# Output projection of a fused attention and expert kernel: three split products, or one product in plain fp32

## The chip, the cores and the metric

The kernel runs on one core of one Trainium2 chip. Its time is the device time of one execution in microseconds. Two runs of the kernel before gave 541.42 and 541.78 us, median 541.6 us. The profiled execution took 541.32 us; its trace covers a span of 539.7 us, from the first to the last instruction.

## The reference

Three layers follow each other. B = 2 sequences of 768 tokens are 1,536 rows; the model width is 512.

```python
x = attention(q, k, v)                      # 1536 x 512
g = x @ w_gate ; val = x @ w_val            # 512 -> 1536
x1 = (silu(g) * val) @ w_out                # 1536 -> 512: the projection
skip = x1 @ w_skip ; e = argmax(x1 @ w_gate2)
out = x1 + gate * (relu(x1 @ w1[e]) @ w2[e])   # rows with skip > 0 only, else x1
```

The change touches the third line, the product of h = silu(g) * val (1536 x 1536) with `w_out` (1536 x 512), and what is made ready for it.

## The kernel before, in words

Everything is fp32 in memory. Where the kernel wants near-fp32 precision from the type fp32r, it splits each operand in two: hi is the operand written as fp32r by ScalarE, lo is the operand less hi, and the product is hi*hi + hi*lo + lo*hi: three matmuls for one product. Elsewhere (attention scores, values, the routing logits, the first expert layer) it hands plain fp32 to the matmul. In the trace a matmul on two plain fp32 operands stands as two MATMUL and two LDWEIGHTS records, a matmul on fp32r as one of each.

The program has four stages.

1. Attention, unrolled, to about 80 us.
2. Gate and value products, 12 slices of 128 hidden columns, each of 14 split products (lines 1538 to 1542). VectorE mixes their results (`mix`) and writes h to `h_sb`, 12 tiles of 128 tokens x 12 slices. Its last steps, for slice 11, come in the order of `MIXES`: h0 (tiles 0 to 5), then c21, m1, h1 (tiles 6 to 11).
3. Projection, 12 tiles of 128 tokens (`rows_of_x1`, lines 1635 to 1656). For each of the 12 slices f the stationary operand is the 128 x 128 piece of h, the moving one the 128 x 512 row block of `w_out`; all accumulate in one PSUM bank, two banks in turn. A tile is cut in two halves of six slices (`tile_of_x1`): after the first half come four transposes of the previous tile's result and two small rank products, after the second the four logits products of the previous tile. ScalarE copies the result out (`copy_rows`), VectorE picks the expert (`choose`, `gates`, `rows_of`), SyncE stores the rows, GpSimd scatters them to the experts' lists.
4. Experts: blocks of 96 rows, first layer in plain fp32 (line 1720), second layer split (lines 1737 to 1739).

Each engine works through its instructions in the order written; `pe.wait_ge` and the like wait on semaphores. Around the change:

- ScalarE's `split_wo` (line 908) writes the hi parts of the 12 row blocks of `w_out`. The lo parts are made by GpSimd (line 729, five of them) and VectorE (line 1277, seven).
- ScalarE's `split_h` (line 901) and VectorE's `split_h` (line 1268) write hi and lo of each tile of h, two instructions each per tile, one or two tiles ahead of TensorE, which waits for the count `h_split`.
- SyncE loads `w_out` to `wo_raw` during the last slice of stage 2 (line 472), and the first experts' weights during stage 3 (lines 477 and 485), some of them behind waits on `h_split`.

Of the kernel before, what the change touches and what calls it, by code (L numbers as in the profile page):

```python
# [7 lines left out]
F32 = mybir.dt.float32  # L8
# [43 lines left out]
WO_POOL = 5  # L52
# [70 lines left out]
def build(nc, qT, kT, v, va, vb, sizes, w_gv, w_out, w_route, w1, w2, out):  # L123
    ctx = ExitStack()
    with ctx:
# [43 lines left out]
        hh_hi = place("hh_hi", (P, 2, FT1, P), 1, 0, F32R)  # L169
        hh_lo = place("hh_lo", (P, 2, FT1, P), 1, 12, F32R)  # L170
# [3 lines left out]
        xres = place("xres", (P, 2, ROW), 0, 50.25)  # L174
        y_sb = place("y_sb", (P, DM), 0, 54.5)
        xgT = place("xgT", (P, KD * ET), 0, 56.5)
        past, more = place("past", (P, MAXT, E - 1), 0, 61), place("more", (P, E, ETILES), 0, 62)
        hg_hi, hg_lo = place("hg_hi", (P, FT2 * ET), 0, 64, F32R), place("hg_lo", (P, FT2 * ET), 0, 68, F32R)

        wo_raw = place("wo_raw", (P, FT1, DM), 1, 0)  # L180
        wo_split = place("wo_split", (P, 2, 2, FT1 // 2, DM), 1, 24, F32R)
# [6 lines left out]
        first_hi, first_lo = place("first_hi", (P, FT1, P), 2, 0, F32R), place("first_lo", (P, FT1, P), 2, 6, F32R)  # L188
# [3 lines left out]
        w2_hi = [place(f"w2_hi{u}", (P, FT2, DM), *home, F32R) for u, home in enumerate(((1, 78.25), (1, 24)))]  # L192
        w2_lo = [place(f"w2_lo{u}", (P, FT2, DM), *home, F32R) for u, home in enumerate(((0, 0), (1, 40)))]
# [117 lines left out]
        wo_hi_made = sem("wo_hi_made")  # L311
        wo_by_pool, wo_by_dve = sem("wo_by_pool"), sem("wo_by_dve")
        x_hi_made = sem("x_hi_made")
        h_hi_made = sem("h_hi_made")
        h_split = sem("h_split")
# [88 lines left out]

        def wo_at(f, part):

            return wo_split[:, f // (FT1 // 2), part, f % (FT1 // 2), :]

        @block.sync
        def _(sp):  # L410
# [117 lines left out]
        def _(pool):  # L528
# [1307 lines left out]
```

## Time and profile before

| | |
|---|---|
| median of 2 runs | 541.6 us |
| profiled execution, its span | 541.32 us, 539.7 us |
| TensorE busy (matmul) | 519.0 us, 96% |
| TensorE weight loads busy | 461.5 us, 86% |
| VectorE, ScalarE, GpSimd busy | 318.3, 214.8, 206.8 us |
| granted TensorE clock, mean | 0.99 |
| share of TensorE in the chain that ended last | 89% |

Busy time of TensorE counts an interval once even where several matmuls are in flight, and a matmul's duration is longer than the distance from its start to the next one's, since they are pipelined. What a matmul costs the engine is that distance, and it is read from the start times of a run of equal instructions.

### The profile page before, as it was taken

How to read it: one execution, taken by the hardware profiler on the slowest of the kernel's cores; microseconds unless marked ns; L12 is line 12 of the kernel's file. 1: busy time of each engine (PE TensorE's matmuls, PEld its weight loads, DVE VectorE, ACT ScalarE, POOL GpSimd, SP SyncE). 2: the span in 40 equal slices, each digit the busy share in tenths (PEclk: the TensorE clock that was granted, in tenths of full speed). 3: DMA queues.
4: the chain of work that ended last, by engine and by line, in shares of the span. 5: the costliest groups of instructions: out<-in, count | busy, mean ns of one | idle time of the engine just before them, and what ended most of it. 6: DMA issues, size and time to landing. Idle time of an engine off the chain costs nothing.

```text
span 539.7 us, 11863 instructions
## 1 busy us (share of the span) xinstructions
PE 519.0 (96%) x3889; PEld 461.5 (86%) x3889; DVE 318.3 (59%) x789; ACT 214.8 (40%) x531; POOL 206.8 (38%) x301
## 2 busy tenths in 40 slices
PE   7999996999999999999989999999999999999993
PEld 5777774999999999999968888888888888888882
DVE  5777777777777777777782343743371515451450
ACT  5778762333333333333643333522231313331440
POOL 7255798966565555555500001010221111111111
PEclk9999999899999999999999999999999999999998
DMA  8996520078777777775635111673319855981511
GB/s 235 299 253 205 173 86 22 2 236 250 232 232 226 237 235 246 232 240 179 234 131 224 56 58 58 234 267 122 108 50 348 315 219 173 339 353 31 185 30 29
DMA packets 42471, 99.69 MB, mean 185 GB/s; under 512 B 2737, under 2 KB 15025, under 8 KB 38337
## 3 DMA queue, kind: packets, MB, share of 16 engines
q1 hardware_dynamic: 24784, 61.24, 32.5%
q10 hardware_dynamic: 15088, 29.87, 18.3%
q0 software_dynamic: 2560, 8.09, 4.5%
q8 instruction: 22, 0.36, 0.3%
q14 instruction: 17, 0.13, 0.1%
HBM read 61.11 MB, written 38.07 MB: 184 GB/s over the span
## 4 chain that ended last, share of the span: by engine, by line
PE 89%; DVE 4%; ACT 2%; issue 1%; DMA 1%; POOL 1%; ACTq 0%; DVEq 0%; POOLq 0%
PE bank L1720 14%; PE bank L1538 11%; PE bank L1542 10%; PE bank L1540 10%; PE bank L1650 6%; PE bank L1654 6%; PE bank L1652 6%; PE bank L1526 4%; PE bank L1737 4%; PE bank L1739 3%; PE bank L1738 3%; PE bank L1503 3%; PE bank L1482 3%; PE bank L1670 2%; ACT probs L812 2%
## 5 line engine op out<-in xcount | busy, mean ns | idle before, releaser
L1538 PE MATMUL bank<-x_blocks,w_blocks 128*128 128x384 f32 x336 | 113.4, 338 | 4.3 <-issue 2.2
L1542 PE MATMUL bank<-x_blocks,w_blocks 128*128 128x384 f32 x336 | 113.2, 337 | 0.0
L1540 PE MATMUL bank<-x_blocks,w_blocks 128*128 128x384 f32 x336 | 113.0, 336 | 0.0
L1720 PEld LDWEIGHTS bank<-xgT,w_sb 128*128 128x128 f32 x704 | 80.4, 192 | 1.4 <-issue 0.4
L1720 PE MATMUL bank<-xgT,w_sb 128*128 128x96 f32 x704 | 80.7, 275 | 0.0
L1538 PEld LDWEIGHTS bank<-x_blocks,w_blocks 128*128 128x128 f32 x336 | 63.8, 190 | 5.1 <-issue 5.1
L1540 PEld LDWEIGHTS bank<-x_blocks,w_blocks 128*128 128x128 f32 x336 | 63.8, 190 | 0.0
L1542 PEld LDWEIGHTS bank<-x_blocks,w_blocks 128*128 128x128 f32 x336 | 63.7, 189 | 0.0
L1650 PE MATMUL bank<-wo_split,hh_hi 128*128 128x512 f32 x132 | 53.7, 407 | 1.8 <-issue 1.8
L642 POOL TENSOR_TENSOR w_blocks<-w_sum,w_blocks 128x256 fp32r<-128x256 f32 x48 | 36.2, 755 | 45.4 <-ACT w_blocks L803 45.4
L736 POOL DMA_INDIRECT expert_rows<-x,row_i x12 | 11.9, 990 | 108.7 <-DVE row_i L1339 100.6
L1654 PE MATMUL bank<-wo_split,hh_lo 128*128 128x512 f32 x132 | 51.8, 393 | 0.0
L1652 PE MATMUL bank<-wo_split,hh_hi 128*128 128x512 f32 x132 | 51.4, 389 | 0.0
L812 ACT ACTIVATE probs<-scores_sb,negmax 128x208 f32<-128x208 f32 (+1 forms) x96 | 42.7, 446 | 16.5 <-DVE negmax L1084 16.5
L994 ACT ACTIVATE hg_hi<-bank 128x384 fp32r<-128x384 f32 x22 | 10.8, 491 | 91.5 <-PE bank L1720 91.5
L1382 DVE SCALAR_TENSOR_TENSOR hg_lo<-bank,hg_hi 128x384 fp32r<-128x384 f32 x22 | 12.2, 556 | 56.2 <-ACT hg_hi L994 56.2
L1084 DVE CUSTOM_DVE_ANT_0 scores_sb<-bank,mask 128x208 f32<-128x208 f32 (+1 forms) x96 | 29.2, 356 | 16.5 <-PE bank L1482 13.5
L1347 DVE TENSOR_TENSOR w_lo<-w_raw,w_hi 128x1024 fp32r<-128x1024 f32 x32 | 37.2, 1218 | 2.6 <-ACT w_hi L959 2.6
L803 ACT ACTIVATE w_blocks<-w_sum 128x256 fp32r<-128x256 f32 x48 | 19.8, 413 | 40.2 <-PE bank L1542 37.2
L1737 PE MATMUL bank<-w_hi,hg_hi 128*96 128x512 f32 x88 | 35.5, 403 | 0.0
L1739 PE MATMUL bank<-w_hi,hg_lo 128*96 128x512 f32 x88 | 34.6, 393 | 0.0
L1738 PE MATMUL bank<-w_lo,hg_hi 128*96 128x512 f32 x88 | 34.5, 392 | 0.0
(197 smaller groups left out, 952.4 us busy)
## 6 DMA issues: line engine op xcount, KB each, us to landing
expert_rows<-pad ACTq DMA_DIRECT2D x10, 2891.2 KB, 14.6
w_raw<-w SPq DMA_DIRECT2D x16, 1024.0 KB, 6.3
w_sb<-w SPq DMA_DIRECT2D x16, 1024.0 KB, 8.9
w_raw<-w_gv SPq DMA_DIRECT2D x12, 512.0 KB, 10.5
va_sb<-v_long SPq DMA_DIRECT2D x10, 512.0 KB, 4.0
vb_sb<-v_tail SPq DMA_DIRECT2D x10, 320.0 KB, 5.3
k_sb<-kT SPq DMA_DIRECT2D x12, 256.0 KB, 5.7
wo_raw<-w_out SPq DMA_DIRECT2D x4, 768.0 KB, 6.3
```

The lines of the kernel that those rows point to most:

```text
L812: nc.scalar.activation(probs[:, qt % 2, h * 2 + u, cols], scores_sb[:, i % 4, cols], ACT.Exp, bias=negmax[:, i % 4:i % 4 + 1], scale=-1.0, ...
L1347: last = nc.vector.tensor_tensor(w2_lo[u][:, f:f + FT2 // 4, :].rearrange("p k c -> p (k c)"), w2_raw[:, p, q:q + FT2 // 4, :].rearrange(" ...
L1538: nc.tensor.matmul(ps, wb[:, p, 0, k, :], xb[:, X_OF[p], 0, k, cols], start=(k == 0 and p in (P1, P6, P5, P7)), stop=False, skip_group_che ...
L1540: nc.tensor.matmul(ps, wb[:, p, 0, k, :], xb[:, X_OF[p], 1, k, cols], start=False, stop=False, skip_group_check=True)
L1542: last = nc.tensor.matmul(ps, wb[:, p, 1, k, :], xb[:, X_OF[p], 0, k, cols], start=False, stop=(k == KD // 2 - 1), skip_group_check=True)
L1650: nc.tensor.matmul(out_ps[u][:, :], h_hi, wo_at(f, 0), start=(f == 0), stop=False, skip_group_check=True)
L1652: nc.tensor.matmul(out_ps[u][:, :], h_hi, wo_at(f, 1), start=False, stop=False, skip_group_check=True)
L1654: last = nc.tensor.matmul(out_ps[u][:, :], h_lo, wo_at(f, 0), start=False, stop=(f == FT1 - 1), skip_group_check=True)
L1720: last = nc.tensor.matmul(ps, w1_sb[u][:, k, fc], xgT[:, k * ET:k * ET + ET], start=(k == 0), stop=(k == KD - 1))
L1737: nc.tensor.matmul(y_ps[0:ET, :], hg_hi[:, hf], w2_hi[u][:, f, :], start=(f == 0), stop=False)
L1738: nc.tensor.matmul(y_ps[0:ET, :], hg_hi[:, hf], w2_lo[u][:, f, :], start=False, stop=False)
L1739: last = nc.tensor.matmul(y_ps[0:ET, :], hg_lo[:, hf], w2_hi[u][:, f, :], start=False, stop=(f == FT2 - 1))
```

## The change

All 144 products of the projection (12 tiles x 12 slices) take `h_sb` and `wo_raw` as they are, in plain fp32: one call to matmul for three. ScalarE's, VectorE's and GpSimd's splits of h and `w_out` go, with the buffers `hh_hi`, `hh_lo`, `first_hi`, `first_lo`, `wo_split` and their semaphores. TensorE now waits for the mixing steps h0 and h1 themselves and for the loads of `w_out`. Its loop over tile pairs is unrolled. `xg`, `xres`, the hidden rows of the experts and the second halves of the expert weights move to other places in on-chip memory; the loads of the experts' weights that waited for `h_split` wait for `rows_in_psum`, and GpSimd's first load of `xg` waits for `products_done`.

```diff
-        xg = place("xg", (P, ROW), 0, 48)
+        xg = place("xg", (P, ROW), 1, 24)
...
-        w2_hi = [place(f"w2_hi{u}", (P, FT2, DM), *home, F32R) for u, home in enumerate(((1, 78.25), (1, 24)))]
-        w2_lo = [place(f"w2_lo{u}", (P, FT2, DM), *home, F32R) for u, home in enumerate(((0, 0), (1, 40)))]
+        w2_hi = [place(f"w2_hi{u}", (P, FT2, DM), *home, F32R) for u, home in enumerate(((1, 78.25), (1, 48)))]
+        w2_lo = [place(f"w2_lo{u}", (P, FT2, DM), *home, F32R) for u, home in enumerate(((0, 0), (0, 48)))]
...
                 if t == NT // 2:
-                    sp.wait_ge(h_split, 2 * 6)
+                    sp.wait_ge(rows_in_psum, 6)
                     load_w1(1)
                 if t == NT // 2 + 1:
-                    sp.wait_ge(h_split, 2 * 8)
+                    sp.wait_ge(rows_in_psum, 8)
                     load_w1(2)
...
-            pool.wait_ge(products_done, LAST + DONE_AT[P5, 1])
-            for f in range(WO_POOL):
-                pool.wait_ge(wo_hi_made, f + 1)
-                nc.gpsimd.tensor_tensor(wo_at(f, 1), wo_raw[:, f, :], wo_at(f, 0).bitcast(F32), ALU.subtract
-                                        ).then_inc(wo_by_pool, 1)
-
...
-            pool.wait_ge(h_split, 2 * (NT - 1))
+            pool.wait_ge(products_done, FT1 * PER_F)
...
-            a.wait_ge(w_lo_made, W_BLOCKS * FT1)
-            a.wait_ge(mixed, FT1 * PER_MIX)
-            split_h(0, 0, first_hi, range(1))
-            a.wait_ge(products_done, LAST + DONE_AT[P6, 1])
-            split_wo(0)
-            split_wo(1)
-            a.wait_ge(mixed, FT1 * PER_MIX + MIX_AT["h0", 0])
-            split_h(0, 0, first_hi, range(1, 2))
-            a.wait_ge(products_done, LAST + DONE_AT[P7, 1])
-            split_wo(2)
-            split_wo(3)
...
-                if (name, j) == ("m0", 1):
-                    split_h(0, 0, first_hi, first_lo, range(1))
-                if (name, j) == ("h0", 1):
-                    split_h(0, 0, first_hi, first_lo, range(1, 2))
-                    d.wait_ge(products_done, LAST + DONE_AT[P3, 1])
-                    split_wo(range(WO_POOL, FT1 * 3 // 4))
-                if (name, j) == ("c21", 1):
-                    split_wo(range(FT1 * 3 // 4, FT1))
...
-            def rows_of_x1(t, u, q, fs=None, hi=None, lo=None):
+            def rows_of_x1(t, u, q, fs=None):
 
                 fs = range(q * FT1 // 2, (q + 1) * FT1 // 2) if fs is None else fs
-                pe.wait_ge(h_split, t * 2 + q + 1)
                 if fs[0] == 0:
 
                     pe.wait_ge(x1_ready, t - 1 + FREE_OUT)
+                    if t % (QT // 2) == 0:
+                        pe.wait_ge(mixed, FT1 * PER_MIX + MIX_AT["h0" if t < QT else "h1", t // (QT // 2) % 2])
                 for f in fs:
...
-                    h_hi = hh_hi[:, u, f, :] if hi is None else hi[:, f, :]
-                    h_lo = hh_lo[:, u, f, :] if lo is None else lo[:, f, :]
-                    nc.tensor.matmul(out_ps[u][:, :], h_hi, wo_at(f, 0), start=(f == 0), stop=False,
-                                     skip_group_check=True)
-                    nc.tensor.matmul(out_ps[u][:, :], h_hi, wo_at(f, 1), start=False, stop=False,
-                                     skip_group_check=True)
-                    last = nc.tensor.matmul(out_ps[u][:, :], h_lo, wo_at(f, 0), start=False,
+                    if t == 0 and f % (FT1 // 4) == 0:
+                        pe.wait_ge(wo_in[f // (FT1 // 4)], 16)
+                    last = nc.tensor.matmul(out_ps[u][:, :], h_sb[:, t, f, :], wo_raw[:, f, :], start=(f == 0),
                                             stop=(f == FT1 - 1), skip_group_check=True)
...
-            pe.wait_ge(mixed, FT1 * PER_MIX + MIX_AT["c12", 0])
             for q in range(2):
-                rows_of_x1(0, 0, q, hi=first_hi, lo=first_lo)
+                rows_of_x1(0, 0, q)
             pe.wait_ge(mixed, FT1 * PER_MIX + MIX_AT["c21", 1])
             tile_of_x1(1, 1, first=True)
-            with pe.Fori(1, NT // 2 - 1) as j:
-                tile_of_x1(j * 2, 0)
-                tile_of_x1(j * 2 + 1, 1)
+            for t in range(2, NT - 2):
+                tile_of_x1(t, t % 2)
```

The first place is TensorE at the end of tile 1's first half and in its second half, before (`hh_hi`, `hh_lo` are the split tile of h, `wo_split` the split `w_out`, `ident` the identity of the transposes). The program lists a matmul once, whether the profile has one record of it or two.

```order
L1650 MATMUL bank<-wo_split,hh_hi 128x512
L1652 MATMUL bank<-wo_split,hh_hi 128x512
L1654 MATMUL bank<-wo_split,hh_lo 128x512
L1663 MATMUL bank<-ident,x_78 128x128 [waits x1T_ready,x1_ready]
L1663 MATMUL bank<-ident,x_78 128x128 x3
L1650 MATMUL bank<-wo_split,hh_hi 128x512 [waits h_split]
```

At the same engine the start of the projection in the changed kernel, tile 0 and the first half of tile 1, reads:

```order
L1566 MATMUL bank<-wo_raw,h_sb 128x512 [waits mixed,wo_in0,x1_ready,wr_in]
L1566 MATMUL bank<-wo_raw,h_sb 128x512 x2
L1566 MATMUL bank<-wo_raw,h_sb 128x512 [waits wo_in1]
L1566 MATMUL bank<-wo_raw,h_sb 128x512 x2
L1566 MATMUL bank<-wo_raw,h_sb 128x512 [waits wo_in2]
L1566 MATMUL bank<-wo_raw,h_sb 128x512 x2
L1566 MATMUL bank<-wo_raw,h_sb 128x512 [waits wo_in3]
L1566 MATMUL bank<-wo_raw,h_sb 128x512 x2
L1566 MATMUL bank<-wo_raw,h_sb 128x512 [waits x1_ready,mixed]
L1566 MATMUL bank<-wo_raw,h_sb 128x512 x5
```

Three rows per slice have become one, and the waits on `h_split` have become waits on the mixing and the loads.

The second place is VectorE between the mixing step h0 and its first work for the routing, before:

```order
L1230 TENSOR_TENSOR h_sb<-m_95,m_97 128x3x128 [waits mixed]
L1268 TENSOR_TENSOR first_lo<-h_sb,first_hi 128x768 [waits h_hi_made]
L1277 TENSOR_TENSOR wo_split<-wo_raw,wo_split 128x512 [waits wo_hi_made,products_done]
L1277 TENSOR_TENSOR wo_split<-wo_raw,wo_split 128x512 [waits wo_hi_made] x3
L1255 TENSOR_TENSOR c_96<-bank,u_93 128x384 [waits products_done] x2
L1277 TENSOR_TENSOR wo_split<-wo_raw,wo_split 128x512 [waits wo_hi_made] x3
L1258 TENSOR_TENSOR m_97<-m_97,c_96 128x384 [waits sig_ready]
```

The same stretch in the changed kernel:

```order
L1180 TENSOR_TENSOR h_sb<-m_92,m_94 128x3x128 [waits mixed]
L1205 TENSOR_TENSOR c_93<-bank,u_90 128x384 [waits products_done] x2
L1208 TENSOR_TENSOR m_94<-m_94,c_93 128x384 [waits sig_ready]
L1180 TENSOR_TENSOR h_sb<-m_94,v_mix 128x3x128 [waits mixed]
L1208 TENSOR_TENSOR m_94<-m_94,c_93 128x384 [waits sig_ready]
```

The step c21 (`c_96`, now `c_93`), for which TensorE waits before tile 1, has lost the lo parts that stood ahead of it.

## Rows read from the trace of the kernel before

**Rows 1.** The page, part 1: busy time, share of the span, instructions.

```profile
PE 519.0 (96%) x3889; PEld 461.5 (86%) x3889; DVE 318.3 (59%) x789; ACT 214.8 (40%) x531; POOL 206.8 (38%) x301
```

**Rows 2.** Windows: stretch, its length, busy us of each engine, PEclk, DMA share, GB/s.

```profile
268.50:276.70 8.20, 8.20 (x38) 6.59 (x36) 8.16 (x13) 4.42 (x9) 0.97 (x1) 1.00 0.00 0
276.70:278.60 1.90, 0.18 (x1) 0.00 (x0) 1.83 (x4) 1.90 (x4) 0.00 (x0) 1.00 0.13 26
278.60:390.00 111.40, 111.36 (x591) 94.14 (x592) 46.77 (x185) 36.73 (x75) 12.03 (x13) 1.00 0.41 152
390.00:400.00 10.00, 9.87 (x69) 8.09 (x68) 8.06 (x30) 4.77 (x7) 1.52 (x2) 1.00 0.14 46
400.00:531.00 131.00, 131.00 (x926) 113.81 (x924) 51.81 (x67) 36.84 (x55) 20.28 (x32) 1.00 0.57 209
```

**Rows 3.** Timeline of TensorE, tile 0 and the idle time behind it: start, us.

```profile
268.52 0.39 PE L1650 MATMUL bank<-wo_split,first_hi 128*128 128x512 f32 x1
276.49 0.39 PE L1654 MATMUL bank<-wo_split,first_lo 128*128 128x512 f32 x1
278.64 0.47 PE L1650 MATMUL bank<-wo_split,hh_hi 128*128 128x512 f32 x1 [1.76 <-issue]
```

**Rows 4.** Timeline of TensorE, one tile in the middle of the projection.

```profile
311.89 0.60 PE L1663 MATMUL bank<-ident,x 128*128 128x128 f32 x4
316.60 0.96 PE L1670 MATMUL bank<-wr_sb,x1T 128*128 128x9 f32 x8
317.42 0.47 PE L1650 MATMUL bank<-wo_split,hh_hi 128*128 128x512 f32 x1
317.73 0.39 PE L1652 MATMUL bank<-wo_split,hh_hi 128*128 128x512 f32 x1
321.63 0.60 PE L1663 MATMUL bank<-ident,x 128*128 128x128 f32 x4
```

**Rows 5.** Timeline of TensorE, plain fp32 score products in attention, cut at three windows.

```profile
20.28 0.41 PE L1482 MATMUL bank<-k_sb,q_sb 64*64 64x208 f32 x4
20.28 0.76 PE L1482 MATMUL bank<-k_sb,q_sb 64*64 64x208 f32 x12
20.28 0.94 PE L1482 MATMUL bank<-k_sb,q_sb 64*64 64x208 f32 x16
```

**Rows 6.** Single lines of the kernel: duration ns min/median/max, first and last start.

```profile
L1482 PE MATMUL bank<-k_sb,q_sb x16: 335/336/387, 20.3 to 20.9; 64*64 64x208 f32 x16
L1526 PE MATMUL bank<-probsT,va_sb x16: 220/222/271, 19.2 to 19.9; 128*64 128x64 f32 x16
L1652 PE MATMUL bank<-wo_split,hh_hi x100: 387/389/395, 299.7 to 379.5; 128*128 128x512 f32 x100
L1540 PE MATMUL bank<-x_blocks,w_blocks x97: 334/334/335, 200.1 to 250.0; 128*128 128x384 f32 x97
```

**Rows 7.** Critical chain in the expert stage: start, us, what.

```profile
414.14 7.12 PE bank L1720 x64
```

**Rows 8.** Lines by form: busy us, mean ns, idle before; TensorE.

```profile
L1720 PEld LDWEIGHTS bank<-xgT,w_sb 128*128 128x128 f32 x704 | 80.4, 192 | 1.4 <-issue 0.4
L1670 PE MATMUL bank<-wr_sb,x1T 128*128 128x9 f32 x88 | 10.5, 247 | 0.0
```

**Rows 9.** Lines by form, VectorE: the split of h.

```profile
L1268 DVE TENSOR_TENSOR hh_lo<-h_sb,hh_hi 128x768 fp32r<-128x768 f32 x22 | 20.0, 953 | 9.6 <-ACT hh_hi L901 9.5
```

**Rows 10.** Timeline of VectorE at the start of the projection.

```profile
266.19 0.56 DVE L1230 TENSOR_TENSOR h_sb<-m,m 128x384 f32<-128x384 f32 x1
270.21 2.49 DVE L1277 TENSOR_TENSOR wo_split<-wo_raw,wo_split 128x512 fp32r<-128x512 f32 x4
272.62 1.01 DVE L1255 TENSOR_TENSOR c<-bank,u 128x384 f32<-128x384 f32 x2
```

**Rows 11.** Timeline of SyncE's queue, and DMA issues: KB each, us to landing.

```profile
256.23 4.02 SPq L472 DMA_DIRECT2D wo_raw<-w_out  x4
wo_raw<-w_out SPq DMA_DIRECT2D x4, 768.0 KB, 6.3
```

More of the change, by code:

```diff
@@ L51 @@
 W_BLOCKS = 7
-WO_POOL = 5
 W_SPLITS = {4: (0, 1), 5: (2, 3), 6: (4,), 7: (5,), 8: (6,)}
@@ L168, in build @@
         all_sum = place("all_sum", (P, 4, KD // 2, P), 2, 26)
-        hh_hi = place("hh_hi", (P, 2, FT1, P), 1, 0, F32R)
-        hh_lo = place("hh_lo", (P, 2, FT1, P), 1, 12, F32R)
         x1 = place("x1", (P, 2, ROW), 1, 72)
         x1T = place("x1T", (P, DM), 1, 76.125)
-        xg = place("xg", (P, ROW), 0, 48)
[L174 to L178, printed above, removed]
+        xg = place("xg", (P, ROW), 1, 24)
+        xres = place("xres", (P, 2, ROW), 1, 26.25)
+        y_sb = place("y_sb", (P, DM), 1, 30.5)
+        xgT = place("xgT", (P, KD * ET), 1, 32.5)
+        past, more = place("past", (P, MAXT, E - 1), 1, 37), place("more", (P, E, ETILES), 1, 38)
+        hg_hi, hg_lo = place("hg_hi", (P, FT2 * ET), 1, 40, F32R), place("hg_lo", (P, FT2 * ET), 1, 44, F32R)
         wo_raw = place("wo_raw", (P, FT1, DM), 1, 0)
-        wo_split = place("wo_split", (P, 2, 2, FT1 // 2, DM), 1, 24, F32R)
         w_raw = place("w_raw", (P, 2, 2, KD, P), 2, 0)
@@ L895, in _ @@
                     slice_of_h(f, u, j * 16 + 16)
-            def split_h(t, u, hi=None, qs=range(2)):
-                for q in qs:
-                    fs = slice(q * FT1 // 2, (q + 1) * FT1 // 2)
-                    nc.scalar.activation((hh_hi[:, u, fs, :] if hi is None else hi[:, fs, :]).rearrange("p f c -> p (f c)"),
-                                         h_sb[:, bass.ds(t, 1), fs, :].rearrange("p a f c -> p (a f c)"),
-                                         ACT.Copy).then_inc(h_hi_made, 1)
-            def split_wo(i):
-                a.wait_ge(wo_in[i], 16)
-                for f in range(i * FT1 // 4, (i + 1) * FT1 // 4):
-                    nc.scalar.activation(wo_at(f, 0), wo_raw[:, f, :], ACT.Copy).then_inc(wo_hi_made, 1)
             copy_p1(FT1 - 1)
             first_sigmoids(FT1 - 1)
-            a.wait_ge(w_lo_made, W_BLOCKS * FT1)
-            a.wait_ge(mixed, FT1 * PER_MIX)
-            split_h(0, 0, first_hi, range(1))
-            a.wait_ge(products_done, LAST + DONE_AT[P6, 1])
-            split_wo(0)
-            split_wo(1)
-            a.wait_ge(mixed, FT1 * PER_MIX + MIX_AT["h0", 0])
-            split_h(0, 0, first_hi, range(1, 2))
-            a.wait_ge(products_done, LAST + DONE_AT[P7, 1])
-            split_wo(2)
-            split_wo(3)
             second_sigmoid(FT1 - 1, 0)
@@ L975, in _ @@
                     copy_rows(t - 1, 1 - u, (j + u) * 16)
-                    split_h(t + 1, 1 - u)
                     exp_logits(t - 2, u)
@@ L1262, in mix @@
                 last.then_inc(mixed, 1)
-            def split_h(t, u, hi=None, lo=None, qs=range(2)):
-                for q in qs:
-                    fs = slice(q * FT1 // 2, (q + 1) * FT1 // 2)
-                    d.wait_ge(h_hi_made, t * 2 + q + 1)
-                    nc.vector.tensor_tensor((hh_lo[:, u, fs, :] if lo is None else lo[:, fs, :]).rearrange("p f c -> p (f c)"),
-                                            h_sb[:, bass.ds(t, 1), fs, :].rearrange("p a f c -> p (a f c)"),
-                                            (hh_hi[:, u, fs, :] if hi is None else hi[:, fs, :]).rearrange(
-                                                "p f c -> p (f c)").bitcast(F32),
-                                            ALU.subtract).then_inc(h_split, 1)
-            def split_wo(fs):
-                for f in fs:
-                    d.wait_ge(wo_hi_made, f + 1)
-                    nc.vector.tensor_tensor(wo_at(f, 1), wo_raw[:, f, :], wo_at(f, 0).bitcast(F32), ALU.subtract
-                                            ).then_inc(wo_by_dve, 1)
             with d.Fori(0, FT1 - 1) as f:
@@ L1360, in _ @@
                     t = j * 2 + u
-                    split_h(t + 1, 1 - u)
                     gates(t - 2, u)
@@ L1365, in _ @@
             for t in range(NT // 2, NT + 1):
-                if t + 1 < NT:
-                    split_h(t + 1, (t + 1) % 2)
                 gates(t - 2, t % 2)
```

21 lines of the change are left out of this document (removed).

## The prediction

> **What bounds the kernel now.** I read the page's busy times first, then the windows by stage, then the timeline of TensorE inside the projection. The busy times show one engine at 96% and the next at 59% [rows 1]. The windows show where that average is made: from 278.6 to 390 us TensorE is busy for 111.36 of 111.40 us, from 400 to 531 us for all of it, and VectorE and ScalarE are busy for less than half of these stretches [rows 2]. The projection begins at 268.52 us, and its only idle time is one gap of 1.76 us behind tile 0 [rows 3]. So in the stage that is changed a microsecond of TensorE is a microsecond of the kernel, and work taken from the other engines is worth at most the 1.8 us of that gap.
>
> The timeline of a middle tile shows how a tile is made up: four transposes at 311.89 and again at 321.63, so 9.74 us per tile, with eight logits records at 316.60 between the halves [rows 4].
>
> **The split products that go.** Tile 0 has 36 wide matmuls with nothing between them; the first starts at 268.52 and the last at 276.49, 35 distances in 7.97 us, 0.2277 us each [rows 3]. The second half of the middle tile gives the same: from the second matmul at 317.73 to the transposes at 321.63 are 17 distances in 3.90 us, 0.229 us [rows 4]. The projection has 12 x 36 = 432 of them: 432 x 0.2277 = 98.4 us, all on the path.
>
> **The plain products that come.** There are 144, and each is two records in the profile, for that is how this kernel's plain fp32 matmuls stand in it: line 1720 has 704 records [rows 8], which are 11 blocks of 32 products, twice. So 288 instructions, 128 rows by 512 columns. No such form is in the trace; the nearest are these.
>
> - The score products in attention, plain fp32, 208 columns, each on a quarter of the array (64 rows, 64 columns). Three cuts of their timeline hold 4, 12 and 16 records that began at 20.28 and last 0.41, 0.76 and 0.94 us [rows 5]. They go four at a time, one on each quarter: from 4 to 12 is two such batches in 0.35 us, from 12 to 16 one in 0.18. From 4 to 16 it is 0.53 / 3 = 0.177 us for a batch, 0.85 ns for a column.
> - The durations of single records say the same in another way. For plain fp32, 222 ns at 64 columns and 336 at 208: 114 / 144 = 0.79 ns per column. For fp32r, 334 at 384 and 389 at 512: 55 / 128 = 0.43 ns per column [rows 6]. So one plain record takes about twice as long per column as one fp32r record. At a granted clock of 1.00 [rows 2], the 2.4 GHz level, these are two periods a column and one.
> - The first expert layer: 64 plain records in 7.12 us, 0.111 us each for 96 columns [rows 7], 1.16 ns per column. But records of 9 columns come eight in the 0.82 us from 316.60 to 317.42, 0.103 us each [rows 4]. So that distance hardly depends on the columns; it is the load of the 128 x 128 weights, whose records fill 80.4 us of that layer [rows 8]. Under a matmul of 512 columns such a load is hidden.
>
> The first two give 0.79 x 512 = 0.405 and 0.85 x 512 = 0.436 us for 512 columns; two periods of the 2.4 GHz clock per column are 0.427. I take 0.43 us, with a few ns for the start of each. The bounds are, below, the distance of an fp32r matmul of the same 512 columns, 0.2277 us; above, 1.16 ns x 512 = 0.593 us.
>
> So 288 x 0.43 = 123.8 us in place of 98.4: **+25.4 us**. A product costs 0.86 us where it cost 0.683.
>
> The first wide matmul behind logits or transposes takes 0.31 us to the next, 0.08 more than the others [rows 4], because the short records ahead of it cannot hide its weight load. That is the same before and after: two per tile, no difference.
>
> **A rule on the same price.** The rows above put the two records of a product at four column periods. The Trainium skill (FP8 and Floating Point Precision, TensorE Precision Notes) says that true fp32 makes four passes through the array, which speaks against replacing three; the durations agree in kind. If each pass cost what an fp32r matmul costs here, a product would be 4 x 0.2277 = 0.911 us, and the sum +32.8 instead of +25.4; that case is a rival below.
>
> **The gap behind tile 0.** TensorE waits there, at 276.7, for the split of tile 1, which ScalarE starts only when the lo parts of `w_out` are done. All that goes. What is left ahead of tile 1 is the step c21; it ran at 272.62, behind 2.49 us of lo parts that go too [rows 10]. Tile 0 itself now ends at 268.5 + 24 x 0.43 = 278.8. The gap closes: **-1.8 us**.
>
> **New waits, at nothing.** Tile 0 now waits for h0 rather than c12: the first h0 ran from 266.19 to 266.75 [rows 10], before TensorE is free at 268.52. It waits for `w_out` itself: the four issues go out between 256.23 and 260.25 and land after 6.3 us, so by about 266.6 [rows 11]. If that load were late by 3 us, TensorE would stand for one. Tiles 3, 6 and 9 wait for mixing steps that are over by 278. Behind a waiting matmul all of TensorE stands, but none of these is late.
>
> SyncE's loads of the second and third experts' weights stand behind the stores of tiles 6 and 7, by when rows of 7 and 8 tiles are in PSUM, so their new waits are satisfied when reached. Its loads ahead of them go out earlier (the first waits for the last mixing step, the second for the end of tile 0). GpSimd's load of `xg` keeps its place behind the scatter of tile 8, and its new wait is long over. In the expert stage TensorE is busy 131.00 of 131 us [rows 2]; nothing there is shortened, nothing waits.
>
> **Splits that go, at nothing.** The lo parts of h are 22 instructions, 20.0 us of VectorE [rows 9], with ScalarE's hi parts beside. They lie beside TensorE, which waits for none of them after tile 1. VectorE is busy 46.8 of 111.4 us [rows 2]. What they gain is slack.
>
> **Sum.** +25.4 - 1.8 = +23.6 us on the profiled execution's 541.3: 564.9 us. The median of the runs is 0.3 above that execution, within what runs differ by, so I predict **565 us**.
>
> **Rivals.**
>
> *A plain record takes one period per column.* Then 512 columns cost the 0.2277 us of the fp32r matmul, 288 x 0.2277 = 65.6 us, and the kernel gains 32.8 + 1.8 = 34.6 us: 507 us. The place is every wide matmul of the projection; it decides the sign as soon as the distance is below (98.4 + 1.8) / 288 = 0.348 us. For it: the batches of four in attention could in truth be pairs in fast succession. Against it: the durations per column, 0.79 against 0.43 ns, and cuts that hold 4, 12 and 16 records, never 6 or 10. By the Trainium skill (TensorE: Matmul & The Clock Gate, Back-to-back issue gap) the gap of a warm matmul is N / 2.4 + 2.5 ns, with no word on the type; for two records of 512 that would be 0.43 us a product and give this same case. The attention rows speak against reading it so, 0.177 us for 208 columns where it has 0.089. Chance 3%.
>
> *Each plain record or pass carries the extra that fp32r matmuls carry.* 512 columns at 0.43 ns are 0.220 us, and the distance is 0.2277, 8 ns more (14 against bare periods). With 14 ns per record a distance is 0.441, the sum +28.6 - 1.8: 568 us. With four full passes, 572.3 us. For it: no row has plain fp32 with 128-column weights behind wide matmuls. Against it: the batches of 208 columns have 4 ns over two periods a column, not 14. Chance 10%, mostly for the near end.
>
> *The weight load is not hidden*, since each product now loads the same piece of h twice and each record reads at the rate of the first expert layer: 0.593 us, +72.4 - 1.8, 612 us. Against it: a load record lasts 0.192 us [rows 8] and would sit under 0.43. Chance 2%.
>
> *The change is slower on TensorE, but relief elsewhere pays for it*, landing within 2%: it would need 13 us of waits inside the projection or behind it, and the windows hold 0.04 us from 278.6 to 390 and 0.13 from 390 to 400 [rows 2]. Chance 2%.
>
> **Chances and range.** The forecast has 83%. Two per cent of the time is 10.8 us, so slower by over 2% is above 552.4: the forecast, the second and the third rival, 95%. Faster by over 2% is the first, 3%; within 2% the last, 2%. Within the forecast the distance may be 0.42 to 0.44, which is 288 x 0.01 = 2.9 us to each side, and contention may add or take 1 us. The range that holds 8 in 10 is 561 to 570; it takes in the near end of the second rival and leaves out the rest.
>
> **What the changed profile would show.** The distance of two wide records in tile 0: 0.42 to 0.44 us if right, 0.23 or 0.59 for the first and third rival. Tiles at a period of 9.74 + 12 x 0.177 = 11.9 us. No idle time of TensorE behind tile 0, tile 0 starting at 268.5. The expert stage as long as before, shifted. I would be wrong if the plain fp32 rate of attention's quarter-array products did not carry over to the full array, or if tile 0 started late for want of `w_out`.

## The result and the profile after

The changed kernel takes 564.6 us (two runs, 564.46 and 564.80), 1.0425 times the kernel before, 95% interval 1.038 to 1.047. It is slower by 23 us, where +23.6 had been forecast. Its profiled execution took 564.8 us and spans 563.2.

First the page of the changed kernel: busy times, the shares of TensorE and others in the chain that ended last, and the wide matmuls (busy us, mean ns | idle before).

```profile
PE 544.6 (97%) x3745; PEld 436.1 (77%) x3745; DVE 292.4 (52%) x758; ACT 191.7 (34%) x495; POOL 200.2 (36%) x296
...
PE 94%; DVE 2%; issue 1%; ACT 1%; POOL 1%; ACTq 0%; DVEq 0%; POOLq 0%
...
L1566 PE MATMUL bank<-wo_raw,h_sb 128*128 128x512 f32 x288 | 129.0, 598 | 0.0
```

TensorE has 144 records fewer than in [rows 1] (432 went, 288 came) and is busy for 25.6 us more. All other engines are relieved: VectorE by 25.9 us, ScalarE by 23.1, GpSimd by 6.6. None of that shows in the time.

The same stretches as in [rows 2]: each has its length, then the busy us of PE, PEld, DVE, ACT and POOL, the granted clock, DMA share, GB/s.

```profile
268.50:279.00 10.50, 10.50 (x30) 5.24 (x29) 3.35 (x7) 1.05 (x2) 0.00 (x0) 1.00 0.51 197
279.00:414.00 135.00, 135.00 (x466) 70.64 (x465) 29.41 (x165) 24.57 (x57) 12.03 (x13) 1.00 0.30 111
414.00:424.00 10.00, 10.00 (x67) 8.01 (x66) 8.32 (x29) 5.12 (x7) 1.51 (x2) 1.00 0.13 46
424.00:555.00 131.00, 130.65 (x922) 113.43 (x920) 51.30 (x66) 36.49 (x55) 20.56 (x32) 1.00 0.57 209
```

TensorE is never idle in the projection; the gap behind tile 0 is gone, and 130.65 of 131 us of the expert stage are filled (131.00 before), at the same granted clock. The list of TensorE's waits from 269 to 555 us is empty.

The timeline of TensorE at the start of the projection, a tile in its middle, and the first expert matmul:

```profile
269.48 15.61 PE L1566 MATMUL bank<-wo_raw,h_sb 128*128 128x512 f32 x36
284.93 0.60 PE L1575 MATMUL bank<-ident,x 128*128 128x128 f32 x4
...
296.56 0.60 PE L1575 MATMUL bank<-ident,x 128*128 128x128 f32 x4
...
308.33 0.60 PE L1575 MATMUL bank<-ident,x 128*128 128x128 f32 x4
...
409.45 1.11 PE L1630 MATMUL bank<-xgT,w_sb 128*128 128x96 f32 x8
```

The 36 records of tile 0 and the first half of tile 1 now stand as one group. The last of them lasts 0.592 us, so 35 distances take 15.61 - 0.592 = 15.02 us, 0.4291 each. From transposes to transposes is 308.33 - 296.56 = 11.77 us, where [rows 4] had 9.74. The difference of 2.03 us is 12 x (2 x d - 3 x 0.2294), where 0.2294 is the fp32r distance in that tile, 3.90 / 17 [rows 4]; it gives d = 0.4287, the same distance in the middle as at the start.

The account of the two profiled executions, in us, with the stages cut at the first wide matmul and at the first matmul of the first expert layer:

| | before | after | difference |
|---|---|---|---|
| to the start of the projection | 268.52 | 269.48 | +0.96 |
| projection | 117.39 | 139.97 | +22.58 |
| from there to the end of the span | 153.8 | 153.8 | 0.0 |

The first line lies in code that the change leaves as it is. Stage 2 starts at 86.78 us before and 87.75 after, and in the profiles of the experiments below anywhere from 86.27 to 88.69: one execution differs from the next by that much there, so the 0.96 us are not the change's.

### The profile page after: what moved, and what is told of

Read it like the earlier page. It is cut to its first block, busy times and chain, and to the rows that moved or that the text cites. A ratio compares the mean times of both kernels' runs of the same rounds, so it can differ in the third digit from the quotient of the medians.

```text
span 563.2 us, 11433 instructions
## 1 busy us (share of the span) xinstructions
PE 544.6 (97%) x3745; PEld 436.1 (77%) x3745; DVE 292.4 (52%) x758; ACT 191.7 (34%) x495; POOL 200.2 (36%) x296
## 4 chain that ended last, share of the span: by engine, by line
PE 94%; DVE 2%; issue 1%; ACT 1%; POOL 1%; ACTq 0%; DVEq 0%; POOLq 0%
PE bank L1566 22%; PE bank L1630 14%; PE bank L1458 10%; PE bank L1460 10%; PE bank L1462 10%; PE bank L1647 4%; PE bank L1649 4%; PE bank L1648 4%; PE bank L1446 4%; PE bank L1423 3%; PE bank L1402 3%; PE bank L1582 2%; PE bank L1416 1%; PE bank L1575 1%; PE bank L1619 1%
## 5 line engine op out<-in xcount | busy, mean ns | idle before, releaser
L1566 PE MATMUL bank<-wo_raw,h_sb 128*128 128x512 f32 x288 | 129.0, 598 | 0.0
L1566 PEld LDWEIGHTS bank<-wo_raw,h_sb 128*128 128x128 f32 x288 | 53.0, 190 | 57.9 <-issue 57.9
L1229 DVE TENSOR_SCALAR computes<-bank 128x1 f32<-128x1 f32 x12 | 1.9, 157 | 70.9 <-PE bank L1582 68.7
## 6 DMA issues: line engine op xcount, KB each, us to landing
w_raw<-w_gv SPq DMA_DIRECT2D x12, 512.0 KB, 10.5
```

The source lines that it names most:

```text
L1566: last = nc.tensor.matmul(out_ps[u][:, :], h_sb[:, t, f, :], wo_raw[:, f, :], start=(f == 0), stop=(f == FT1 - 1), skip_group_check=True)
```

## The experiments

Three theories were to be told apart first. **Theory A**, that of the prediction: TensorE's stream of columns is the whole story; a plain fp32 record takes two periods of the 2.4 GHz clock per column and next to nothing besides, and relief of the other engines is worth nothing. **Rival B**: each record carries a fixed extra as an fp32r matmul does (0.2277 us against 0.2133 for 512 bare periods, 14 ns). **Rival C**: something of the 23 us is made elsewhere, or was given back elsewhere. The ratios are to the kernel before, timed beside each.

### Two matmuls of 256 columns for one of 512

```diff
-                    last = nc.tensor.matmul(out_ps[u][:, :], h_sb[:, t, f, :], wo_raw[:, f, :], start=(f == 0),
+                    for c in (slice(0, DM // 2), slice(DM // 2, DM)):
+                        last = nc.tensor.matmul(out_ps[u][:, c], h_sb[:, t, f, :], wo_raw[:, f, c], start=(f == 0),
```

> The changed kernel with each plain fp32 product of 512 columns cut into two of 256, same stationary piece of h: 576 records where there were 288, half as wide. If a record costs two clock periods per column and a few ns (0.4286 us at 512 columns in the changed kernel), the distance at 256 columns is about 0.2155 us, 576 x 0.2155 = 124.1 us against 123.4, and the kernel takes 565 us (564.6 + 0.7). If instead a record's cost does not depend on its columns, because the load of its weights or a fixed cost bounds it, 576 x 0.4286 = 246.9 us and the kernel takes 688 us. If the distance has a large fixed part beside the columns, it lands between.

Measured: 604.0 us, ratio 1.116 (1.114 to 1.118), which fits none of the figures expected. But the projection took 409.02 - 268.33 = 140.69 us, only 0.72 more than in the changed kernel; the time is lost behind it. Two lines of its page, matmuls by form:

```profile
L1567 PE MATMUL bank<-wo_raw,h_sb 128*128 128x256 f32 x576 | 129.8, 382 | 0.0
...
L1631 PE MATMUL bank<-xgT,w_sb 128*128 128x96 f32 x896 | 102.6, 275 | 0.0
```

The first expert layer has 896 records, 14 blocks of 64, where it had 704, 11 blocks. Both halves of a PSUM bank began with `start`, and the second `start` made the first slice's part of the left half vanish: the logits came out different, the rows fell to the experts in another way, and three more blocks were needed. The total is 604.0 - 564.6 = 39.4 us above the changed kernel's, so with the 0.7 of the projection taken off, a block costs 12.9. So this kernel leaves a twelfth of the sum of half the columns out, and its total says nothing on the question; its projection does. The same with one `start` per bank:

```diff
-                        last = nc.tensor.matmul(out_ps[u][:, c], h_sb[:, t, f, :], wo_raw[:, f, c], start=(f == 0),
+                        last = nc.tensor.matmul(out_ps[u][:, c], h_sb[:, t, f, :], wo_raw[:, f, c], start=(f == 0 and c.start == 0),
```

> The run with two 256-column halves again, with the accumulation begun once per bank (only the left half of slice 0 clears it), so that the first slice's part of the left half is kept and the experts get the same blocks of rows as in the changed kernel. Two periods per column: 576 records at the 0.216 us that the first version of this run showed are 124.4 us against 123.4, and the kernel takes 564.6 + 0.7 = 565.3 us. A cost per record would give 688 us.

Measured: 564.5 us, ratio 1.043 (1.040 to 1.046), as the uncut changed kernel. Its timeline, the records of tile 0 and half of tile 1, and the durations of its line, ns min/median/max:

```profile
268.55 15.70 PE L1567 MATMUL bank<-wo_raw,h_sb 128*128 128x256 f32 x72
```

```profile
L1567 PE MATMUL bank<-wo_raw,h_sb x576: 378/379/463, 268.6 to 409.0; 128*128 128x256 f32 x192
```

71 distances take 15.70 - 0.379 = 15.32 us, 0.2158 each. Two distances and two widths give the price apart: (0.4291 - 0.2158) / 256 = 0.833 ns per column, exactly two periods of 2.4 GHz, and 0.2158 - 0.2133 = 2.5 ns for a record. The projection takes 409.24 - 268.55 = 140.69 us, again 0.72 more than uncut, and 288 more records of 2.5 ns are 0.72. Rival B wanted 14 ns each, 4 us; it is out.

The Trainium skill (TensorE: Matmul & The Clock Gate, Back-to-back issue gap) has N / 2.4 + 2.5 ns for an isolated warm matmul of N columns. With 2N in the place of N it gives 0.2158 and 0.4292 us for these records, and the trace agrees to 0.1 ns, though these stand in a stream, for which the section expects less than the formula; as it stands it would be short by half.

### The splits put back on ScalarE and VectorE, with nobody waiting for them

```diff
+            def split_h(t):
+                for q in range(2):
+                    fs = slice(q * FT1 // 2, (q + 1) * FT1 // 2)
+                    a.wait_ge(dummy_lo, t * 2 + q)
+                    nc.scalar.activation(dummy[:, fs, :].rearrange("p f c -> p (f c)"),
+                                         h_sb[:, bass.ds(t, 1), fs, :].rearrange("p a f c -> p (a f c)"),
+                                         ACT.Copy).then_inc(dummy_hi, 1)
```

VectorE has the like, a subtraction behind `dummy_hi`, 22 instructions on each engine for tiles 1 to 11.

> The changed kernel with the splits of h given back to ScalarE and VectorE as idle work: tiles 1 to 11 are copied to a scratch buffer and subtracted there, 22 instructions of about 0.84 us on ScalarE and 22 of about 0.95 us on VectorE at the places where they stood; TensorE reads neither and waits for neither. If the relief of these engines is worth nothing in the projection, the kernel takes 564.6 us again, within 1. If part of the price of plain fp32 was paid back by freeing them, or if they slow TensorE's reads, it takes longer: at most 20 us of VectorE's work could appear, 584 us.

Measured: 563.7 us, ratio 1.042 (1.040 to 1.044). A line by form of VectorE, the window of the projection, and TensorE's first group in it:

```profile
L1300 DVE TENSOR_TENSOR dummy<-h_sb,dummy 128x768 fp32r<-128x768 f32 x22 | 20.1, 953 | 10.9 <-ACT dummy L889 10.8
```

```profile
268.00:407.00 139.00, 139.00 (x444) 69.94 (x443) 49.01 (x181) 38.99 (x74) 11.05 (x12) 1.00 0.32 119
```

```profile
267.45 15.61 PE L1597 MATMUL bank<-wo_raw,h_sb 128*128 128x512 f32 x36
```

The 20.1 us on VectorE are there again, as in [rows 9], and the projection lasts 407.42 - 267.45 = 139.97 us, the same to the hundredth. The relief of these engines is worth nothing while TensorE is the bound. Rival C is out on this side.

Behind the projection the trace of this run has one wait more. TensorE's waits from 268 to 555 us, a list that is empty in the changed kernel:

```profile
PE bank L1650 <- DMA xg<-expert_rows: 1.1, 1, 1.1
```

TensorE stands 1.1 us in the expert stage for a load of the experts' rows, and from the first expert matmul to the end of the span are 154.8 us instead of 153.8. The total doesn't show it, since the stages ahead ran 2.0 us shorter in this execution. That the returned work delays this load is likely but not shown. In the kernel before, the stretch is 153.8 as well, so the change itself gained nothing there.

### Fewer products in the kernel before

If TensorE alone were the bound in the kernel before, taking matmuls out should return each at 0.2277 us. Two kernels do this. The first leaves out hi of h times lo of `w_out`, the second both products with a lo part; their outputs lack those terms.

```diff
                     nc.tensor.matmul(out_ps[u][:, :], h_hi, wo_at(f, 0), start=(f == 0), stop=False,
                                      skip_group_check=True)
-                    nc.tensor.matmul(out_ps[u][:, :], h_hi, wo_at(f, 1), start=False, stop=False,
-                                     skip_group_check=True)
                     last = nc.tensor.matmul(out_ps[u][:, :], h_lo, wo_at(f, 0), start=False,
```

> The kernel before with the middle one of the three fp32r products of each slice left out (hi of h with lo of w_out), its waits kept: 288 wide matmuls instead of 432. If each costs 0.2277 us on the path, tiles 1 to 11 save 11 x 12 x 0.2277 = 30.1 us, and tile 0 saves nothing, since what follows waits for the splits until 278.6 as before: 541.6 - 30.1 = 511.5 us. If VectorE or ScalarE become the bound at a period of 7.0 us per tile, the kernel saves less, 515 to 530 us. Together with the changed kernel this gives the price of a plain product in fp32r passes: by my reading 0.857 / 0.2277 = 3.8 passes.

> The kernel before with two of the three fp32r products of each slice left out (all that has a lo part), its waits kept: 144 wide matmuls. The run with two products showed TensorE waiting for the copy of a tile's result, which waits for the scatter that frees its buffer. If that chain now bounds the projection, the two half tiles that lie in it get 1.4 us shorter each in every two tiles, and the kernel gains about 1.4 us per tile on the run with two products: 533.7 - 14 = 520 us, 517 to 526. If TensorE's matmuls were still the bound, 11 x 12 x 0.2277 = 30.1 us less: 503.6 us.

Measured: 533.7 us with two products, ratio 0.986 (0.984 to 0.988), and 532.5 us with one, ratio 0.984 (0.981 to 0.987). The first 144 matmuls return 7 to 8 us of 32.8, the next 144 one. Both expectations fell. The waits from 280 to 370 us of the kernel with two products, of TensorE and then of ScalarE (us in total, times, longest):

```profile
PE bank L1661 <- ACT x L931: 13.9, 7, 3.0
```

```profile
ACT x L931 <- POOLq L739: 42.6, 7, 7.7
```

The window of the same stretch, two products and then one:

```profile
280.00:370.00 90.00, 75.99 (x367) 61.49 (x368) 41.26 (x151) 31.98 (x62) 7.97 (x8) 0.92 0.44 169
```

```profile
280.00:370.00 90.00, 60.34 (x261) 47.61 (x260) 40.73 (x157) 32.23 (x64) 9.04 (x10) 0.80 0.44 167
```

TensorE's transposes wait for ScalarE's copy of the tile (`copy_rows`), and the copy waits for GpSimd's scatter, which must have read the buffer first. So a cycle runs beneath TensorE's work: copy, split of the next tile, routing, scatter, buffer free, copy. Its period in the kernel with two products is 8.5 to 10.5 us per tile, from copy to copy. The kernel before already shows it, ScalarE's waits from 280 to 380 us:

```profile
ACT x L931 <- POOLq L739: 39.8, 8, 6.9
```

There it is hidden: a tile of TensorE takes 9.74 us, and the cycle is shorter on average (9.4 us in the kernel with two products, eight turns from 298 to 374 us). At the closest the copy ends at 369.21 us, 1.0 us before the transposes that need it; ScalarE and TensorE:

```profile
368.61 0.60 ACT L931 ACTIVATE x<-bank 128x512 f32<-128x512 f32 x1 [6.87 <-POOLq L739]
```

```profile
370.21 0.60 PE L1663 MATMUL bank<-ident,x 128*128 128x128 f32 x4
```

In the changed kernel, from 270 to 410 us, the same copy waits for TensorE instead:

```profile
ACT x L888 <- PE bank L1566: 33.7, 7, 9.2
ACT x L888 <- POOLq L720: 10.2, 2, 5.2
```

A second loss comes with the waits. Stretches of the kernel with two products:

```profile
305.00:310.00 5.00, 2.29 (x12) 1.67 (x12) 0.34 (x1) 3.09 (x4) 0.00 (x0) 0.85 0.17 67
310.00:315.00 5.00, 5.00 (x22) 4.19 (x23) 2.72 (x13) 0.93 (x4) 0.96 (x1) 0.81 0.13 50
...
340.00:345.00 5.00, 2.33 (x11) 1.56 (x9) 2.88 (x5) 0.59 (x2) 0.51 (x1) 1.00 0.61 254
345.00:350.00 5.00, 4.94 (x18) 4.04 (x19) 2.74 (x10) 2.15 (x6) 0.54 (x1) 0.66 0.83 275
```

In both places 2.7 us of idle time of TensorE are followed by some us at the 1.2 GHz level. TensorE is busy there, but does less; two wide matmuls from the second:

```profile
347.96 0.63 PE L1650 MATMUL bank<-wo_split,hh_hi 128*128 128x512 f32 x1
348.39 0.63 PE L1652 MATMUL bank<-wo_split,hh_lo 128*128 128x512 f32 x1
```

They are 0.43 us apart, where the same matmul costs 0.2277 at the 2.4 GHz level. Over the 90 us the mean of 0.92 is worth at most 0.08 x 90 = 7 us. With the 14.0 us of idle time that is up to 21 of the some 25 us that were missing.

### Tile 1's split earlier, in the kernel before

This is meant to take away the gap of 1.76 us [rows 3] and leave the rest; the price is that the mixing steps m1 and h1 come later.

```diff
             split_wo(3)
+            a.wait_ge(wo_by_pool, WO_POOL)
+            a.wait_ge(wo_by_dve, 1)
+            split_h(1, 1)
...
-            a.wait_ge(wo_by_pool, WO_POOL)
             a.wait_ge(wo_by_dve, FT1 - WO_POOL)
-            split_h(1, 1)
...
                     split_wo(range(FT1 * 3 // 4, FT1))
+                    d.wait_ge(wo_by_dve, FT1 - WO_POOL)
+                    split_h(1, 1)
...
-            split_h(1, 1)
```

> The kernel before with one thing changed: tile 1 of h is split earlier, its hi parts on ScalarE right behind the hi parts of w_out and its lo parts on VectorE right behind the last lo parts of w_out, ahead of the mixing steps m1 and h1. By my reading of the gap of 1.76 us behind tile 0 as a wait for this split, the gap goes and the kernel takes 539.8 us, ratio 0.997. If the gap is a wait for something else (the mixing step c21, the logits banks), it stays and the kernel takes 541.6 us; if delaying m1 and h1 makes a later tile wait, up to 543.5.

Measured: 539.9 us, ratio 0.998 (0.997 to 0.999). TensorE's timeline where the gap was:

```profile
277.59 0.39 PE L1656 MATMUL bank<-wo_split,first_lo 128*128 128x512 f32 x1
277.82 0.39 PE L1652 MATMUL bank<-wo_split,hh_hi 128*128 128x512 f32 x1
```

The last matmul of tile 0 and the first of tile 1 are 0.23 us apart. The projection is 384.99 - 269.62 = 115.37 us, 2.02 less. So the gap's term is a real 1.8 to 2.0 us, and a third product per slice, with no gap, is what the plain kernel has to be held against: 139.97 against 115.37.

### Where the cycle is held up

The next runs ask why two products don't return more. In all of them the same terms are left out as above (hi of h times lo of `w_out`). The theories: the rank products' place on TensorE, the exponential's place on ScalarE, and the splits' place in the queues of ScalarE and VectorE. In the kernel before, `split_h` of the next tile stands behind `copy_rows` on ScalarE and so starts only when the buffer is free, and on VectorE ahead of `gates` and `rows_of`, which give the scatter its row numbers.

Rank products after the third slice, together with the early split of tile 1:

```diff
-                rows_of_x1(t, u, 0)
-                columns_of_x1(t - 1, 1 - u)
+                rows_of_x1(t, u, 0, range(3))
...
+                rows_of_x1(t, u, 0, range(3, FT1 // 2))
+                columns_of_x1(t - 1, 1 - u)
```

> The run with two of three products (hi of h with lo of w_out left out), with tile 1 split earlier and the two rank products moved from behind the transposes to behind the third slice of a tile. If the chain from a tile's logits through the ranks and the scatter to the release of its buffer bounds the projection, the ranks come 1.8 us earlier in a cycle of two tiles: 0.9 us per tile for some 9 tiles, 8 us, and 2 us from the early split: 533.7 - 10 = 524 us. If the landing of the scatter or of other DMAs sets the period whatever the ranks do, 531 to 533 us.

Measured: 532.8 us, ratio 0.986 (0.982 to 0.990). Not the ranks.

The exponential ahead of the copy and the split, alone and then with the ranks and the early split:

```diff
+                    exp_logits(t - 2, u)
                     copy_rows(t - 1, 1 - u, (j + u) * 16)
                     split_h(t + 1, 1 - u)
-                    exp_logits(t - 2, u)
...
```

> The run with two of three products (hi of h with lo of w_out left out), and ScalarE's routing exponential of tile t-2 moved from behind the copy and split of tile t-1 and t+1 to ahead of them. Reading of the last two runs: with fewer matmuls the period of 8.5 to 10.5 us per tile is set on ScalarE's queue: the copy waits for the scatter of the tile before last, the exponential stands behind the copy and two split instructions of 0.8 us, and the next scatter waits for the exponential. If so, the period falls to 7.0 to 7.7 us and the kernel from 533.7 to 510 to 520 us. If the landing of the scatter beside the weight loads sets it, it stays above 530.

> The same with tile 1 split earlier and the rank products behind the third slice as well (two of three products, hi of h with lo of w_out left out). If the exponential's place was what hid the gain of these two moves, TensorE is the bound again: 541.2 less 30.1 for the matmuls and less 1.5 to 2 for the gap, 509.5 us, 507 to 514. If the chain is set elsewhere, about 530 as without it.

Measured: 533.1 us, ratio 0.984 (0.980 to 0.989), and 532.1 us, ratio 0.982 (0.979 to 0.985). In both, the gain that was expected did not come; the second figure of each expectation, the one without it, is what was met. The trace of the second shows the whole cycle; from three answers of its timeline, ScalarE, VectorE and GpSimd:

```profile
324.88 0.60 ACT L934 ACTIVATE x<-bank 128x512 f32<-128x512 f32 x1 [3.05 <-POOLq L739]
325.37 1.57 ACT L901 ACTIVATE hh_hi<-h_sb 128x768 fp32r<-128x768 f32 x2
...
333.21 0.60 ACT L934 ACTIVATE x<-bank 128x512 f32<-128x512 f32 x1 [2.61 <-POOLq L739]
```

```profile
326.24 1.83 DVE L1269 TENSOR_TENSOR hh_lo<-h_sb,hh_hi 128x768 fp32r<-128x768 f32 x2 [4.02 <-ACT hh_hi L901]
...
328.96 0.16 DVE L1342 TENSOR_TENSOR row_i<-row_sum,trash 128x1 int32<-128x1 f32 x1
```

```profile
329.93 0.96 POOL L736 DMA_INDIRECT expert_rows<-x,row_i  x1 [7.72 <-DVE row_i L1342]
```

The copy at 324.88 lets the split's hi part go at 325.37; VectorE stands for it for 4.02 us and makes the lo part till 328.07; only then come the row numbers, the scatter at 329.93, and the next copy at 333.21: a turn of 8.33 us, the quickest of this trace. From copy to scatter it is 5.05 us here, and 5.0 to 5.2 in the other turns from 298 us on; what makes these up to 10.3 us long is the scatter's way to its landing, up to 5.4 us where it is 3.1 here.

Of the two parts the queues hold the first. The copy should not be ahead of the split, nor the split ahead of the routing. Against the kernel just read, the same in the loops over the last tiles:

```diff
                     exp_logits(t - 2, u)
-                    copy_rows(t - 1, 1 - u, (j + u) * 16)
+                    a.wait_ge(rows_in_psum, t)
                     split_h(t + 1, 1 - u)
+                    copy_rows(t - 1, 1 - u, (j + u) * 16)
...
-                    split_h(t + 1, 1 - u)
                     gates(t - 2, u)
                     rows_of(t - 2, u)
+                    split_h(t + 1, 1 - u)
```

> The last run (two of three products, hi of h with lo of w_out left out) with the splits of h taken out of the cycle that its trace shows: copy of a tile, hi split behind it on ScalarE, lo split behind that on VectorE, ranks' row numbers behind that, scatter, release of the buffer, next copy, 8.4 us in all. ScalarE now splits ahead of the copy, VectorE behind the row numbers. If this queue order set the period, it falls towards the 7.0 us of TensorE and the kernel to 510 to 516 us from 532. If the scatter's landing beside the weight loads sets it, it stays above 528.

Measured: 524.2 us, ratio 0.967 (0.965 to 0.970), between the theory's figure and the rival's. Waits from 280 to 370 us, TensorE's and ScalarE's, the window, and two copies in the timeline of ScalarE:

```profile
PE bank L1665 <- ACT x L934: 9.4, 3, 4.0
```

```profile
ACT x L934 <- POOLq L739: 9.6, 3, 4.0
```

```profile
280.00:370.00 90.00, 80.33 (x423) 64.42 (x422) 44.94 (x179) 36.27 (x72) 13.96 (x13) 0.96 0.50 183
```

```profile
319.69 0.57 ACT L934 ACTIVATE x<-bank 128x512 f32<-128x512 f32 x1
...
326.76 0.58 ACT L934 ACTIVATE x<-bank 128x512 f32<-128x512 f32 x1
```

Copy to copy is 7.07 us here, which is TensorE's own time for a tile of two products (9.74 - 12 x 0.2277 = 7.01), and no wait stands before either copy. The queue order was a cause, worth 8 us. Three waits for the scatter are left, 9.4 us of TensorE in all.

What holds those three back is the landing, the rival of the expectation. The time from issue to landing of the scatter issued at 287.3 us, of the four from 298.0 to 320.8, and of the three from 329.9 to 346.7 (us min/median/max):

```profile
DMA to landing us min/median/max: 9.7/9.7/9.7
DMA to landing us min/median/max: 3.2/3.6/4.0
DMA to landing us min/median/max: 6.9/7.6/8.7
```

And the windows of the first scatter's landing and of quick ones:

```profile
287.00:297.00 10.00, 6.75 (x36) 5.19 (x34) 5.07 (x18) 2.37 (x5) 2.00 (x1) 1.00 0.72 254
306.00:325.00 19.00, 19.00 (x105) 15.48 (x104) 10.09 (x38) 8.29 (x16) 3.87 (x3) 1.00 0.22 83
```

The waiting copies begin at 297.08, 336.95 and 355.58 us, each within 0.2 us of the landing of a late scatter. All four late ones fall where SyncE's loads of the experts' weights are under way (four of 1,024 KB issued from 279.6 us, two each at 327.8, 338.0 and 346.9), with the DMA engines 72 to 81% busy. That the landing ends the waits is shown; that the loads delay it goes by this coincidence, for no run moved them. So with the queues in order a part of the rival holds as well, and the next step would be to place those loads elsewhere.

Last, this order with all three products, a kernel that leaves nothing out:

```diff
                     nc.tensor.matmul(out_ps[u][:, :], h_hi, wo_at(f, 0), start=(f == 0), stop=False,
                                      skip_group_check=True)
+                    nc.tensor.matmul(out_ps[u][:, :], h_hi, wo_at(f, 1), start=False, stop=False,
+                                     skip_group_check=True)
```

> The same order of work with all three products, so a complete kernel: TensorE's tile of 9.74 us is longer than any cycle seen on the other engines, so only the gap behind tile 0 goes, as in the run that split tile 1 early: 539.8 us, ratio 0.997. More gain would mean that the other engines did hold TensorE back in the kernel before.

Measured: 540.3 us, ratio 0.997 (0.995 to 0.998). With three products the cycle is hidden anyway, and only the gap behind tile 0 is gained, as by the early split alone. Of the kernels that compute the whole sum these two are the fastest, by 0.2 to 0.3%; they are not told apart.

## Why the prediction was right, point by point

- **TensorE is the bound in the projection.** Right, and shown: idle for nothing of it after the change, and 20 us of work on VectorE with as many instructions on ScalarE, put beside it, leave its length the same.
- **432 split products go, 98.4 us.** Taken from starts in the trace of before. The kernels with fewer products show that this could not have been cashed in as a saving: there 144 of them returned 7 us of 32.8. Here it was a term of an exchange in which TensorE stayed the bound, and so it held.
- **288 records at 0.43 us.** The distance is 0.4291; the bounds had been 0.2277 and 0.593. The choice rested on attention's quarter-array products and on the durations per column, and both carried over to the full array: 0.833 ns per column, where they gave 0.85 and 0.79.
- **The gap behind tile 0 closes, -1.8 us.** Right; alone it is worth 2.0 us in the profile and 1.0 to 1.5 in the medians.
- **New waits at nothing.** Right; TensorE's list of waits is empty. Two rows of VectorE's timeline of the changed kernel show the nearest ones, the first h0 and the second c21:

```profile
267.15 0.56 DVE L1180 TENSOR_TENSOR h_sb<-m,m 128x384 f32<-128x384 f32 x1
269.68 0.56 DVE L1205 TENSOR_TENSOR c<-bank,u 128x384 f32<-128x384 f32 x1 [0.44 <-PE bank L1462]
```

  The first h0 is done 1.8 us before the first wide matmul at 269.48. The second c21 is over at 270.24, 3.4 us earlier than in [rows 10], and tile 1 starts 24 x 0.429 = 10.3 us behind 269.48. The last load of `w_out` lands at 268.3 (7.5 us from its issue, where the prediction took 6.3); it is needed first at slice 9 of tile 0.
- **Splits that go, at nothing, "What they gain is slack".** Right for this change. What the prediction did not say is how thin the cover was: the kernel before had 39.8 us of waits for the scatter under TensorE's tiles, at the closest 1.0 us from holding TensorE, and at 7 us per tile instead of 9.74 they come to the surface. Nor did it look behind the projection, where in the run with the splits put back TensorE waits 1.1 us for a load.
- **The sum.** +23.6 forecast for the projection, +22.6 measured. The distances hold most of that 1.0: at 0.4291 the plain products cost 123.6 instead of 123.8, and the split ones had 0.2294 rather than 0.2277 behind tile 0, 36 x 0.2277 + 396 x 0.2294 = 99.0 instead of 98.4. With the gap that is 123.6 - 99.0 - 1.8 = +22.8. The prediction saw both distances and took the smaller for all. The profiled executions lie 23.5 apart, with the 0.96 us of the stages ahead, which is spread between executions; so the forecast's closeness to the total is in part luck.

Of the rivals, one period per column would have given distances of 0.2277, the load in the open 0.593; neither is there. The extra per record is 2 to 3 ns and not 14. The Trainium skill's four passes (FP8 and Floating Point Precision, TensorE Precision Notes) agree with what the trace shows, two records of two periods per column; priced as four fp32r matmuls they would have given 0.455 us per record, and it is 0.429.

## What to carry to other kernels

On this chip three fp32r products (3 x 0.2277 us) are cheaper than one in plain fp32 (2 x 0.4291) for 512 columns; by these prices the plain form could pay only where the splits themselves, or what waits for them, set the end, a case that no run here has, so read first whether TensorE is idle in the stage. Before costing the removal of work from the bounding engine, look for waits on other engines that it hides, add up the cycle through buffers and queues, and take the saving only down to that cycle's period, with the transfers in it as long as they take beside the other loads. In an engine's queue, work that others wait for belongs ahead of work that can wait, and a copy that must wait for a buffer belongs behind both.

## What the runs showed of the hardware

- A plain fp32 matmul is two records, each of two periods of 2.4 GHz per column and about 2.5 ns: 0.2158 us for 256 columns, 0.4291 for 512. The 14 ns that an fp32r matmul of 512 columns has over its bare periods are no cost of a matmul as such.
- A `start` on one half of a PSUM bank costs the other half what it had gathered: 604.0 us and 14 expert blocks with two, 564.5 us and no more blocks than before with one. The Trainium skill (PSUM — Partial Sum Buffer, The four PSUM rules) says the same: the first matmul of a group clears the written marks of the whole bank, so the other group's next product overwrites its sum. The runs agree in this effect.
- Idle times of 2.7 us of TensorE were followed by stretches at the 1.2 GHz level (means of 0.81 and 0.66 over 5 us), so that with one product per slice the mean from 280 to 370 us was 0.80. A matmul of 512 columns in fp32r costs 0.43 us there instead of 0.2277. Here taking matmuls out also slowed those that were left.
- The scatter of a tile's rows landed 3.2 to 4.0 us after its issue where the DMA engines were 15 to 22% busy, and 6.9 to 9.7 us after it where they were 72 to 81% busy with loads of weights.
